# Mixture-of-experts routing rewritten: choice and places by scans on rows, three of four batches placed during attention

## The reference

```python
def _attn_ref(q, k, v):                      # 4 batches, 8 heads, 576 tokens, 64 columns
    q_d = q.reshape(B, H, Sd, 4, D).mean(axis=3)      # k_d, v_d alike
    out_up = np.repeat(sm_attn(q_d, k_d, v_d), 4, axis=2)
    mask = np.abs(pos[:, None] - pos[None, :]) < 4
    scores = np.where(mask, scale * q @ k.T, -1e9)
    return out_up + softmax(scores) @ v

def _moe_ref(x, w_gate, w_local, w1, w2):    # x 4 x 576 x 512, E = 8, F = 1024
    logits = np.einsum('bsd,de->bse', x, w_gate)
    local_gate = 1 / (1 + np.exp(-np.einsum('bsd,de->bse', x, w_local)))
    for b in range(B):
        prev_e = -1
        for s in range(S):
            fresh_e = int(np.argmax(logits[b, s]))
            e = fresh_e if s == 0 or local_gate[b, s] < 0.5 else prev_e
            prev_e = e
            p = softmax(logits[b, s])
            h = np.maximum(x[b, s] @ w1[e], 0.0)
            out[b, s] = p[e] * (h @ w2[e])

def _moe2_ref(x, w_tok1, w_tok2, w_ch1, w_ch2):   # token mixer, then channel mixer
    u = x + (np.maximum(x.T @ w_tok1, 0) @ w_tok2).T
    return u + np.maximum(u @ w_ch1, 0) @ w_ch2
```

## Time and profile before

| | |
|---|---|
| median of 3 unprofiled runs | 949.73 us (949.61 to 949.76) |
| the profiled execution: its own time | 952.06 us |
| its span, first to last instruction | 950.2 us |
| PE busy | 854.1 us, 90% of the span |
| DVE, ACT, POOL busy | 455.8, 346.8, 222.5 us |
| mean granted TensorE clock | 0.971 of 2.4 GHz |
| attention, up to the last `xT` | 234 us |
| routing, to the first expert matmul | 234 to 279.7 us |
| experts, to the last slot's copy | 279.7 to 571 us |
| token and channel mixer | to 950 us |

### The profile page before, as it was taken

How to read it: one execution, slowest core, us unless ns; L and a number is a source line. 1 busy time by engine, 2 the same in 40 slices (tenths; PEclk the granted TensorE clock), 3 DMA queues, 4 the chain that set the end, 5 groups by cost and what they waited for, 6 DMA issues and landing times.

```text
span 950.2 us, 13283 instructions
## 1 busy us (share of the span) xinstructions
PE 854.1 (90%) x4424; PEld 710.9 (75%) x4425; DVE 455.8 (48%) x880; ACT 346.8 (36%) x866; POOL 222.5 (23%) x344
## 2 busy tenths in 40 slices
PE   5889898777139999999999995999999999999998
PEld 3666667654128888878887884898999988999997
DVE  6896968877355436153565526512112343121211
ACT  5576666744214525253554425111111211111110
POOL 6886867752011221211221210000000000000000
PEclk9999999999659999999999997999999999999999
DMA  9657786400425346162665334000101010000000
GB/s 158 118 101 181 148 197 133 112 7 1 165 94 187 123 142 210 44 209 79 206 212 188 116 127 156 1 1 12 55 1 67 1 67 1 1 34 1 34 1 34
DMA packets 94157, 88.44 MB, mean 93 GB/s; under 512 B 63197, under 2 KB 69011, under 8 KB 94111
## 3 DMA queue, kind: packets, MB, share of 16 engines
...
...
## 4 chain that ended last, share of the span: by engine, by line
PE 71%; DVE 14%; DMA 5%; POOL 3%; issue 3%; ACT 2%; SPq 1%; POOLq 0%; ACTq 0%; DVEq 0%
PE bank L1474 16%; PE bank L1476 16%; PE bank L1475 16%; PE bank L1524 4%; PE bank L1531 4%; PE bank L1525 4%; DMA stage<-in_moe_w 2%; PE bank L1515 2%; DVE xT L1049 2%; PE bank L1355 2%; DVE aT L1027 2%; DVE kB L992 2%; DVE nm L1005 1%; PE bank L1382 1%; PE bank L1482 1%
## 5 line engine op out<-in xcount | busy, mean ns | idle before, releaser
L1257 DVE SCALAR_TENSOR_TENSOR h2l<-bank,h2h 128x384 fp32r<-128x384 f32 x72 | 40.2, 558 | 190.0 <-ACT h2h L930 190.0
L930 ACT ACTIVATE h2h<-bank 128x384 fp32r<-128x384 f32 x72 | 35.4, 492 | 229.7 <-PE bank L1476 229.7
L1474 PE MATMUL bank<-uTh,W 128*128 128x384 f32 x288 | 98.1, 340 | 0.0
L1475 PE MATMUL bank<-uTl,W 128*128 128x384 f32 x288 | 97.5, 338 | 0.0
L1476 PE MATMUL bank<-uTh,W 128*128 128x384 f32 x288 | 97.1, 337 | 0.0
L1476 PE MATMUL bank<-W,h2l 128*128 128x512 f32 x216 | 84.5, 391 | 0.0
L1474 PE MATMUL bank<-W,h2h 128*128 128x512 f32 x216 | 84.3, 390 | 0.0
L1475 PE MATMUL bank<-W,h2h 128*128 128x512 f32 x216 | 84.1, 389 | 0.0
L1206 DVE TENSOR_TENSOR W<-stage,W 128x1024 fp32r<-128x1024 f32 x56 | 66.6, 1221 | 26.1 <-ACT W L886 26.1
L886 ACT ACTIVATE W<-stage 128x1024 fp32r<-128x1024 f32 x56 | 57.7, 1054 | 53.6 <-DVE ysb L1224 29.0
L1474 PE MATMUL bank<-W,xTh 128*128 128x512 f32 x184 | 75.4, 410 | 1.6 <-DVE xTl L1184 1.6
...
## 6 DMA issues: line engine op xcount, KB each, us to landing
stage<-in_moe_w SPq DMA_DIRECT2D x56, 512.0 KB, 4.6
...
```

What stands on the lines that cost most here:

```text
L930: act.activation(dst, bank[bk][:, 0:width], ACT.Relu).then_inc(relu_hi, 1)
L1257: dve.scalar_tensor_tensor(dst, bank[bk][:, 0:width], 0.0, hi.bitcast(F32), ALU.max, ALU.subtract).then_inc(bank_free, 1)
L1474: pe.matmul(ps, ah, bh, start=first, stop=False)
L1475: pe.matmul(ps, ah, bl, start=False, stop=False)
```

## The change

Logits are made per token tile: 96 tokens (stationary) by 10 columns (moving), 12 matmuls for half a batch, placed at units 3 and 5 of an even block, rows at 2, 4, 6, 7, 8. A token's mark is a row of 8 values, +1 at its fresh expert and -1 elsewhere if it chooses afresh, 0 everywhere if it keeps; six small matmuls turn the marks to one row for each batch and expert. On that row one scan (`run_on`) carries the choice along and one (`count`) numbers the tokens of each expert; with the start of each batch's and expert's share that is the token's place. Nothing goes through memory. Each expert gets 18 columns of its own in the map, so places don't depend on the counts of other experts; a small table `tab` turns the number of a slot into its column. Batches 0 to 2 (`early`) are marked, scanned and placed in blocks 6 and 7 and their one-hot columns made there (steps `RA` + 6 to + 20, with `RA` = 54 the first step of block 6); batch 3 (`last`) after attention. Expert 0's weight splits move from blocks 6 and 7 to blocks 3 to 6, four in each. `stage` now shares its memory with the early one-hots, so the loads of expert 1 wait for `inverted`. The token mixer's loads move between those of experts 2 and 3 on SP's queue, ACT's split of them ahead of expert 6. The shares of the chosen experts (`shares`, 96 x 24) go through `p_dr` to `prob`: ACT issues the store behind `x_hi(0)`, SP the load after the last expert's weights.

```diff
 def side_work(g):
+    if g - RA in (9, 10, 13, 14):
+        work.append(("route", 0, (9, 10, 13, 14).index(g - RA)))
...
-        if 2 <= u < 2 + LT:
-            work.append(("rows", b, u - 2))
-        if u >= 7:
-            work.append(("logits", b, u - 7))
+        if u in (2, 4, 6, 7, 8):
+            work.append(("rows", b, (2, 4, 6, 7, 8).index(u)))
+        if u in (3, 5):
+            work.append(("logits", b, (3, 5).index(u)))
...
 def split_work(g):
-    if hb == NHB - 2 and u in (1, 2, 4, 5, 6, 8):
-        return [(1, 2, 4, 5, 6, 8).index(u)]
-    if hb == NHB - 1:
-        return [6 + u] if u < 8 else [14, 15]
+    if 3 <= hb < 7 and u in (1, 2, 5, 6):
+        i = (1, 2, 5, 6).index(u)
+        return [2 * (hb - 3) + i % 2 + CPE * (i // 2)]
...
-            sp.wait_ge(fkT_done, 1)
-            sp.dma_start(fk_dr.rearrange("a (t p) -> (a t) p", p=P), fkT[:, :]).then_inc(fk_out, 16)
-            sp.wait_ge(fk_out, 16)
-            sp.dma_start(fl[:, :, :], fk_dr.rearrange("a (b s) -> b a s", b=B)).then_inc(fl_in, 16)
-            sp.wait_ge(scanned, 1)
-            sp.dma_start(e_dr.rearrange("(b s) -> b s", b=B), eseq[:, :]).then_inc(e_out, 16)
-            sp.wait_ge(e_out, 16)
-            sp.dma_start(eT[:, :], e_dr.rearrange("(t p) -> t p", p=P)).then_inc(eT_in, 16)
...
+            sp.wait_ge(inverted, 1)
             sp.wait_ge(hi_done, CPE + NST)
+            with sp.Fori(1, 3) as e:
+                load_expert(e)
+            sp.dma_start(raw1[:, 0:4, :], w_tok1[0:4 * P, :].rearrange("(k p) c -> p k c", p=P)).then_inc(tok_in, 16)
...
+            with sp.Fori(3, E) as e:
+                load_expert(e)
+            sp.wait_ge(p_out, 16)
+            sp.dma_start(prob[:, :], p_dr.rearrange("(t p) -> p t", p=P), allow_slow_non_contiguous=True
+                         ).then_inc(p_in, 16)
...
+            pool.wait_ge(gidx_done, 1)
+            pool.wait_ge(x_stored, 1)
+            pool.indirect_dma_start(out=xg[:, :], out_offset=None, in_=x_dr,
+                                    in_offset=bass.IndirectOffsetOnAxis(ap=gidx[:, 0:1], axis=0)
+                                    ).then_inc(gathered, 16)
...
+            x_hi(0)
             act.wait_ge(route_done, 1)
-            x_hi(0)
+            act.wait_ge(prob_done, 1)
+            act.dma_start(p_dr.rearrange("(k p) -> p k", p=QP), shares[:, :, :].rearrange("p b t -> p (b t)"),
+                          allow_slow_non_contiguous=True).then_inc(p_out, 16)
...
+            def run_on(w, r):
+                step(dve.tensor_tensor_scan(r.seq[:, :], r.xr[:, :], r.xr[:, :], 0.0, ALU.is_ge, ALU.is_le))
+
+            def count(w, r):
+                step(dve.tensor_tensor_scan(r.cum[:, :], r.seq[:, :], r.seq[:, :], 0.0, ALU.add, ALU.max))
+
+            def place(w, r):
+                dve.scalar_tensor_tensor(r.pos[:, :], r.cum[:, :], r.base[:, 0:1], r.seq[:, :], ALU.add, ALU.mult
+                                         ).then_inc(pos_done[w], 1)
...
+            def hot_columns(w, r, k):
+                t, b = k // r.nb, k % r.nb + (B1 if w else 0)
+                for src, dst in ((id_hi, r.hot_hi), (id_lo, r.hot_lo)):
+                    dve.tensor_scalar(dst[:, k, :], col_row[0:QP, :], r.col[:, k:k + 1], src[:, b, t:t + 1],
+                                      ALU.is_equal, ALU.mult).then_inc(hot_done[w], 1)
...
+                if g == 11:
...
+                    run_on(0, early)
+                if g == 12:
+                    count(0, early)
+                    dve.sem_inc(cum_done[0], 1)
...
+                if 15 <= g < 21:
+                    for k in range(3 * (g - 15), 3 * (g - 14)):
+                        hot_columns(0, early, k)
...
+            choose(1, last)
...
+            run_on(1, last)
+            count(1, last)
+            place(1, last)
...
+            lanes(1, last, bank[4][0:QP, 0:KT])
+            for k in range(KT):
+                dve.tensor_scalar(last.hot_lane[:, k, :], lane_row[0:QP, :], last.lane[:, k:k + 1], None, ALU.is_equal
+                                  ).then_inc(hot_lane_done[1], 1)
+                hot_columns(1, last, k)
...
-                for kc in range(KD):
-                    mm = pe.matmul(side_bank(what)[0:E2, 0:LGC], wg[:, kc, :], xT[:, kc, c * LGC:(c + 1) * LGC],
-                                   start=(kc == 0), stop=(kc == KD - 1))
+                for t in range(3):
+                    cols = slice((3 * c + t) * QP, (3 * c + t + 1) * QP)
+                    for kc in range(KD):
+                        mm = pe.matmul(side_bank(what)[0:QP, t * E2:(t + 1) * E2], xT[:, kc, cols], wg[:, kc, :],
+                                       start=(kc == 0), stop=(kc == KD - 1))
...
+            def places(ps, chosen, r):
+
+                for t in range(KT):
+                    cols = slice(t * QP, (t + 1) * QP)
+                    pe.matmul(ps[0:QP, t * r.nb:(t + 1) * r.nb], r.pos[:, cols], of_batch[0:r.m, 0:r.nb],
+                              start=True, stop=True)
+                    mm = pe.matmul(chosen[:, t * r.m:(t + 1) * r.m], r.seq[:, cols],
+                                   ident[0:r.m, 0:r.m], start=True, stop=True)
```

561 lines of the change are left out of this document (352 added, 209 removed).

## The result

The changed kernel is slower: 968.02 us median (965.17 to 969.83, 4 runs) against 949.67 (949.49 to 949.76, 4 runs), ratio 1.0179, 95% interval 1.0163 to 1.0196. The prediction was 943.7 (936 to 950). The profiled execution took 967.19 with a span of 965.5, 15.3 above the span before.

What follows compares the result with a forecast made beforehand. It took VectorE to bound attention's odd blocks, TensorE the experts and mixer, and a barely overlapping chain the routing. Routing -19.7, attention +12.9, expert 0 +0.8: -6.0 on 949.73 gives 943.7 us, range 936 to 950.

Steps and rivals of the forecast that it cites:

- Block 7 and tail: +3.9: Last attention block to last xT: splits leave, scans, placing and one-hots arrive; +3.9 us, between 1 and 7.
- The marks and their neighbours: Block 6: about eleven small routing operations, 3.4 us of VectorE, counted as 2.0; with two splits fewer, +1.2 us.
- The tail's 18 one-hots against three splits: Attention's tail, 222 to 234 us: 18 hot columns replace three splits, +0.5 us.
- TensorE's clock: First expert's first 5 us: granted 0.50 (1.2 GHz) kept as before; 2 to 3 us less if 2.4 GHz at once.
- a logits group: Attention: 24 instructions moving 10 columns and loading 96 take 2.3 us instead of 2.11; +1.2 us over six.
- Rival 2: Logits and places: weight loads don't overlap, each load-and-move pair takes 0.163 us; 16.4 us more, 960 us; chance 0.11.
- Splits: Four weight splits each in blocks 3 to 6: blocks 3 and 5 pay 6.2 us together, block 4 1.6; block 6 saves 0.8.
- The gap: Last xT to first expert matmul: from 45.7 to 26.0 us, saving 19.7 (17 to 22).
- My 3.66: Routing gap: the gather's time, taken as 3.66 us as in the kernel before.
- Expert 0: First expert: +0.8 us for ScalarE's p_dr store issue and its traffic; weight loads now start later.
- Rival 3: First expert: p_dr's small writes and late stage loads hold its chunks, 5 us instead of 0.8; 948 us; chance 0.10.
- the loop's sensitivity: Attention: what would above all make the forecast wrong is a loop answering more to VectorE's order than its sum; no size.

Runs made afterwards that it cites:

- hots_gap: Changed kernel with 24 of the 36 early one-hot columns made after the last attention unit: 960.2 us, ratio 1.012 to the kernel before.
- no_pad: even_late with logits matmuls that move 10 columns again instead of 64: 959.3 us, ratio 1.010 to the kernel before.
- stage_late: Changed kernel with expert 1's first weight loads issued only once the first gather has landed: 970.9 us, ratio 1.019 to the kernel before.
- before_splits: Kernel before with only the 16 weight splits moved from blocks 6 and 7 to blocks 3 to 6: 951.9 us, ratio 1.000.
- even_late: Changed kernel, one-hots in gap, placement spaced, 64-column logits, raw0 loads earlier, share store and expert 1 loads later, blocks 4 and 6 splits in units 3-6: 953.7 us.
- gap_order: even_late with seven early one-hot calls in VectorE's waits, last marks turned between row transposes, early inversion split: 945.6 us, ratio 0.995 to the kernel before.

## Why the prediction was wrong

- **The sum of VectorE in block 7 and the tail** ("Block 7 and tail: +3.9", 1 to 7) is the step that failed most: +12.1. The sum had 2.4 us more work for VectorE and 1.5 of waiting; measured are 8.9 and 3.2. I can name 6.1 of the 6.5 us of work that it missed. A one-hot I put at 0.20 us; six without a wait take 1.6 us (238.83 to 240.42), and the 36 cover 9.4 us instead of 7.4: 2.0. The marks and their neighbours, 1.4, land here and not in block 6. VectorE comes 1.8 us late out of block 6 (it still has a unit's operations from 213.4 to 215.2). The tail's 18 one-hots against three splits I put at +0.5, where my own prices make 1.4: 0.9. That the stretch follows this work hots_gap shows: 24 one-hots out of it, 5.4 us less, 0.23 each. The waiting goes with the clock of 0.77 and I can't part the two.
- **TensorE's clock** I considered for the first expert alone. Shown: the logits' short moves bring it down in block 2 (seven executions against seven), and beside the other amendments they cost 6 to 8 us (no_pad). How much of the 18 us of the changed kernel they are is not shown; padding them there did not move the median. The 2.3 us that I gave a logits group was right (2.18); the cost is in the instructions behind it. Rival 2 looked at the same edit and had the wrong mechanism: the loads do overlap, each lasts 0.16 us and the pairs come 0.09 apart. Waits for ScalarE or VectorE go with other falls (102, 163.5, 228 us); that they cause them is argued only.
- **Splits:** sum right (before_splits), its division among the blocks not, and not the same in two executions.
- **The gap:** of the missing 6.8 us the first gather is 3.4 (shown by stage_late), the last logits, rows and marks at 1.2 GHz some 3.0 (10.3 us to the copied marks instead of 7.3; read from rows, not tried alone). My 3.66 came from a gather that ran alone; I had counted that SP's loads start late and not that they start with it. The one-hots for the last batch, 0.21 each with POOL's share on VectorE, were priced well.
- **Expert 0:** +0.8 forecast, +1.4 measured from its first matmul to the end. Rival 3 had the right store and mostly the wrong victim: it held the second gather (2.5 us of TensorE's time); for the chunks ScalarE waited 1.5 us.
- **Right:** the logits' own time, the trips through memory gone, the choice and the scans by their rows, and the loop's sensitivity named as what would make it wrong. What it named, the one-hots between a probability copy and the next maximum, was not tried apart from their sum.
- **Open:** where the falls of one variant come is not settled; two executions of one program (it is the same up to block 6 in even_late and gap_order) have block 1 at 24.0 and 28.0 us, and that the wider scatter of the changed kernel comes from them is argued only.
